# Block means of the values by VectorE sums over features-first values and one transpose, in an attention kernel with two feed-forward stages

## What is computed

```python
k_sum = k.reshape(B, H, nb, 32, D).max(axis=3)       # nb = 24 blocks of 32 tokens
v_sum = v.reshape(B, H, nb, 32, D).mean(axis=3)
scores_l = scale * q @ k^T, kept where |i - j| < 16
scores_s = scale * q @ k_sum^T + log(32)
a = softmax(concat(scores_l, scores_s))
out = a @ concat(v, v_sum)
```

## Time and profile before

| | |
|---|---|
| median of 3 runs | 642.89 us (641.2 to 645.67) |
| span of the profiled execution | 640.1 us |
| TensorE busy (matmul) | 621.3 us, 97% |
| VectorE busy | 446.0 us, 70% |
| ScalarE busy | 262.2 us, 41% |
| GpSimd busy | 145.3 us, 23% |

### The profile page before, as it was taken

One profiled execution on the slowest core, in us unless ns is written; L12 is line 12 of the kernel. 1 busy time (PEld: TensorE's weight loads), 2 busy tenths in 40 slices (PEclk: granted clock), 3 DMA queues, 4 the chain that ended last, 5 costly groups with the idle time before them and its releaser, 6 DMA issues.

```text
span 640.1 us, 9485 instructions
## 1 busy us (share of the span) xinstructions
PE 621.3 (97%) x3072; PEld 519.2 (81%) x3072; DVE 446.0 (70%) x864; ACT 262.2 (41%) x553; POOL 145.3 (23%) x146
## 2 busy tenths in 40 slices
PE   5999998999999999999999989999999999999996
PEld 5999996888888888888888867778888888888885
DVE  4555557966534333345666589999999999999996
ACT  2556553111013111131111374556676666766663
POOL 5344424000003000030000084642222222222220
PEclk9999999999999999999999989999999999999998
DMA  9786744500000000002323310000010000100001
GB/s 215 182 213 179 187 121 175 209 1 0 1 0 0 0 0 0 0 1 98 99 98 100 99 33 0 1 1 0 2 66 0 0 0 0 66 1 0 1 0 66
DMA packets 27096, 35.46 MB, mean 55 GB/s; under 512 B 1984, under 2 KB 19392, under 8 KB 27072
## 3 DMA queue, kind: packets, MB, share of 16 engines
q1 hardware_dynamic: 24672, 33.96, 17.9%
q10 hardware_dynamic: 2400, 1.18, 0.8%
HBM read 30.80 MB, written 3.15 MB: 53 GB/s over the span
## 4 chain that ended last, share of the span: by engine, by line
PE 57%; DVE 34%; issue 6%; ACT 1%; DVEq 1%; DMA 1%; SPq 0%
PE bank L488 21%; PE bank L546 20%; DVE ratio L953 9%; PE bank L443 8%; DVE numer L935 5%; DVE ratio L947 5%; DVE numer L933 5%; DVE ratio L942 5%; DVE hhi L960 4%; PE bank L474 2%; PE bank L461 2%; PE bank L453 2%; PE bank L561 1%; DMA qblk<-qT 1%; DVE hlo L964 0%
## 5 line engine op out<-in xcount | busy, mean ns | idle before, releaser
L488 PE MATMUL bank<-xhi,whi 128*128 (+1 forms) x384 | 150.1, 391 | 1.2 <-DVE wlo L841 1.2
L488 PE MATMUL bank<-xlo,whi 128*128 (+1 forms) x384 | 149.9, 390 | 0.0
L488 PE MATMUL bank<-xhi,wlo 128*128 (+1 forms) x384 | 149.6, 390 | 0.0
L405 POOL TENSOR_TENSOR denom<-denom,habs 128x512 f32<-128x512 f32 (+1 forms) x49 | 62.3, 1271 | 253.0 <-ACT denom L713 253.0
L642 ACT ACTIVATE hsq<-bank 128x512 f32<-128x512 f32 x48 | 28.7, 598 | 218.6 <-PE bank L488 218.6
L488 PEld LDWEIGHTS bank<-xhi,whi 128*128 128x128 f32 x384 | 72.2, 188 | 16.4 <-DVE wlo L841 1.4
L488 PEld LDWEIGHTS bank<-xhi,wlo 128*128 128x128 f32 x384 | 72.3, 188 | 15.1
L488 PEld LDWEIGHTS bank<-xlo,whi 128*128 128x128 f32 x384 | 72.3, 188 | 14.9
L561 PE MATMUL bank<-whi,hhi 128*128 128x512 f32 x192 | 76.8, 400 | 6.5 <-DVE hlo L964 6.5
L561 PE MATMUL bank<-whi,hlo 128*128 128x512 f32 x192 | 76.1, 396 | 0.0
L561 PE MATMUL bank<-wlo,hhi 128*128 128x512 f32 x192 | 75.9, 395 | 0.0
(11 more groups left out here) (69 smaller groups left out, 917.4 us busy)
## 6 DMA issues: line engine op xcount, KB each, us to landing
wraw<-w SPq DMA_DIRECT2D x32, 512.0 KB, 3.8
kraw<-kT SPq DMA_DIRECT2D x8, 384.0 KB, 6.5
qblk<-qT SPq DMA_DIRECT2D x16, 192.0 KB, 3.1
vnat<-v SPq DMA_DIRECT2D x8, 384.0 KB, 5.4
vwin<-v SPq DMA_DIRECT2D x8, 384.0 KB, 4.7
out<-osb SPq DMA_DIRECT2D x12, 256.0 KB, 2.1
vwin<-v SPq DMA_DIRECT2D x16, 88.0 KB, 4.5
vwin<-vsum ACTq DMA_DIRECT2D x8, 144.0 KB
```

What stands on the lines that cost most here:

```text
L405: g.tensor_tensor(denom[:, i, cols], denom[:, i, cols], habs[:, i, cols], ALU.mult).then_inc(q_done, 1)
L488: last = mm(hps[j % 2][:, :], W[a][:, j, kt * P:(kt + 1) * P], X[b][:, kt, bass.ds(CH * c, CH)], start=k == 0, stop=k == 3 * KT - 1)
```

## The change

The means are no longer made by matmuls. The values are loaded a second time features-first, as the keys are (`vT`, 128 features on the partitions, 768 tokens in a row), into `vraw` in place of `vnat`. VectorE sums each 32 tokens with a reduction (`block_sum`) into `vred`, a tile of 128x24. TensorE transposes `vred` once, and ScalarE scales by 1/32 as it copies the result out of PSUM. Both tiles, `vred` and `vsum`, now start at partition 0. The matrix `mean` and what builds it on GpSimd are gone.

`block_sum` stands right behind each `block_max`: whole (24 blocks) for the first two blocks at the start, and in thirds (8 blocks) for block (it+1, s) in the three steps of block (it, s).

```diff
@@ sync
-        def load_vnat(it, s):
-            sp.dma_start(vnat[s][:, :, :], pick(v, it, s).rearrange("(n p) c -> p n c", p=P)).then_inc(vn_in[s], 16)
+        def load_vraw(it, s):
+            sp.dma_start(vraw[s][:, :], pick(vT, it, s)).then_inc(vr_in[s], 16)
...
                 load_q(it + 1, s)
                 load_vwin(*((it, 1) if s == 0 else (it + 1, 0)))
-                sp.wait_ge(vsum_done, n + 1)
-                load_vnat(it + 1, s)
+                sp.wait_ge(vred_done, GPB * (n + 1))
+                load_vraw(it + 1, s)
@@ gpsimd: memset and two affine_select of mean removed
@@ tensor, summary(it, s)
-            pe.wait_ge(vn_in[s], 16 * (it + 1))
+            pe.wait_ge(vred_done, GPB * (n + 1))
             pe.wait_ge(vsum_copied, n)
-            for i in range(S // P):
-                last = mm(vps[KW:COLS, 0:P], mean[:, i, :], vnat[s][:, i, :], start=i == 0, stop=i == S // P - 1)
-            last.then_inc(vsum_done, 1)
+            nc.tensor.transpose(vps[0:NBLK, 0:P], vred[s][:, :], ident[:, :]).then_inc(vsum_done, 1)
@@ scalar, copy_summary
-            a.copy(vsum[s][KW:COLS, :], vps[KW:COLS, 0:P]).then_inc(vsum_copied, 1)
+            a.activation(vsum[s][:, :], vps[0:NBLK, 0:P], ACT.Copy, scale=1.0 / BLOCK).then_inc(vsum_copied, 1)
@@ vector
+        def block_sum(it, s, part, parts, first=False):
+
+            n = B * it + s
+            if part == 0:
+                dve.wait_ge(vr_in[s], 16 * (it + 1))
+                if not first:
+                    dve.wait_ge(vsum_done, n - 1)
+            blocks = NBLK // GPB
+            lo, hi = blocks * part, blocks * (part + parts)
+            d.tensor_reduce(vred[s][:, lo:hi],
+                            vraw[s][:, BLOCK * lo:BLOCK * hi].rearrange("p (n t) -> p n t", t=BLOCK),
+                            AX.X, ALU.add).then_inc(vred_done, parts)
...
                     block_max(it + 1, g // GPB, g % GPB, 1)
+                    block_sum(it + 1, g // GPB, g % GPB, 1)
...
         block_max(0, 0, 0, GPB, first=True)
+        block_sum(0, 0, 0, GPB, first=True)
         make_mask()
...
         block_max(0, 1, 0, GPB, first=True)
+        block_sum(0, 1, 0, GPB, first=True)
         masked(2, 2)
```

More of the change, by code:

```diff
@@ L67, in done, with build @@
     return credits + i + 1
-def build(nc, qT, kT, v, w1, w2, coef_a, coef_b, out):
+def build(nc, qT, kT, vT, v, w1, w2, coef_a, coef_b, out):
     base = 16512
@@ L112, in build @@
     half = FT // 2 * SLOT * 4
-    qblk, kraw, kwin, vwin, vnat = [], [], [], [], []
+    qblk, kraw, kwin, vwin, vraw = [], [], [], [], []
     for s in range(B):
@@ L119, in build @@
         vwin.append(area(f"vwin{s}", [COLS, NW, P]))
-        vnat.append(area(f"vnat{s}", [P, S // P, P]))
+        vraw.append(area(f"vraw{s}", [P, S]))
         assert area.offset <= (W_HI, W_LO)[s] + 2 * half
@@ L126, in build @@
     ident = area("ident", [P, P])
-    mean = area("mean", [P, S // P, NBLK])
-    vsum = [area(f"vsum{s}", [P, P]) for s in range(B)]
+    vred = [area(f"vred{s}", [P, NBLK]) for s in range(B)]
+    vsum = [area(f"vsum{s}", [NBLK, P]) for s in range(B)]
     ksum = [area(f"ksum{s}", [P, NBLK]) for s in range(B)]
@@ L156, in build @@
     k_in = [sem(f"k_in{s}") for s in range(B)]
-    vn_in = [sem(f"vn_in{s}") for s in range(B)]
+    vr_in = [sem(f"vr_in{s}") for s in range(B)]
     vw_in = [sem(f"vw_in{s}") for s in range(B)]
@@ L174, in build @@
     dve_turn = sem("dve_turn")
+    vred_done = sem("vred_done")
     vsum_done = sem("vsum_done")
@@ L256, in _ @@
         load_q(0, 0)
-        load_vnat(0, 0)
+        load_vraw(0, 0)
         sp.wait_ge(cleared, 3)
@@ L261, in _ @@
         load_q(0, 1)
-        load_vnat(0, 1)
+        load_vraw(0, 1)
         sp.dma_start(ca[:, :], coef_a.partition_broadcast(P)).then_inc(coef_in, 16)
@@ L302, in _ @@
         g.memset(ident[:, :], 0.0).then_inc(pool_step, 1)
-        g.memset(mean[:, :, :], 1.0 / BLOCK).then_inc(pool_step, 1)
         for i in range(2):
             g.memset(band[i][:, :], 0.0).then_inc(pool_step, 1)
-        pool.wait_ge(pool_step, 4)
+        pool.wait_ge(pool_step, 3)
         g.affine_select(out=ident[:, :], in_=ident[:, :], compare_op=ALU.not_equal, fill=1.0, base=0,
                         pattern=[[-1, P]], channel_multiplier=1).then_inc(consts, 1)
-        g.affine_select(out=mean[:, :, :], in_=mean[:, :, :], compare_op=ALU.is_ge, fill=0.0, base=0,
-                        pattern=[[P, S // P], [-BLOCK, NBLK]], channel_multiplier=1).then_inc(pool_step, 1)
         for i in range(2):
@@ L316, in _ @@
         pool.wait_ge(consts, 1)
-        pool.wait_ge(pool_step, 7)
-        g.affine_select(out=mean[:, :, :], in_=mean[:, :, :], compare_op=ALU.is_ge, fill=0.0, base=BLOCK - 1,
-                        pattern=[[-P, S // P], [BLOCK, NBLK]], channel_multiplier=-1).then_inc(consts, 1)
+        pool.wait_ge(pool_step, 5)
         for i in range(2):
@@ L526, in attention @@
                     output(it, s, gi, G, g % 2)
-        pe.wait_ge(consts, 4)
+        pe.wait_ge(consts, 1)
         pe.wait_ge(cleared, 3)
@@ L636, in spread_summary @@
             act.dma_start(vwin[s][KW:COLS, :, :],
-                          vsum[s][KW:COLS, :].unsqueeze(1).to_broadcast([NBLK, NW, P])).then_inc(vsum_in[s], 16)
+                          vsum[s][:, :].unsqueeze(1).to_broadcast([NBLK, NW, P])).then_inc(vsum_in[s], 16)
         def relu(n, i):
@@ L776, in make_mask @@
         def make_mask():
-            dve.wait_ge(consts, 4)
+            dve.wait_ge(consts, 3)
             for h in range(2):
@@ L1008, in by_query @@
         return np.ascontiguousarray(features_first(t).reshape(PAIRS, B, P, NW, QW).swapaxes(3, 4))
-    arrays = {"qT": by_query(q), "kT": features_first(k), "v": tokens_first(v),
+    arrays = {"qT": by_query(q), "kT": features_first(k), "vT": features_first(v), "v": tokens_first(v),
               "w1": slots(moe_w_in, moe_w_out), "w2": slots(moe2_w_in, moe2_w_out),
```

## The result

The changed kernel takes 659.75 us (median of 4 runs, 659.52 to 660.97), the kernel before 642.05 us in the same comparison. The ratio is 1.0266, with a 95% interval of 1.0232 to 1.0301: slower by 17.7 us by the medians. The profiled execution took 659.79 us, with a span of 658.0, so 1.8 us lie around the span.

A forecast was written before the change was run, and what follows sets the result against it. TensorE was taken to bound attention; the values' late load would stall blocks: 2.7 + 5 x 3.02 - 1.27 = +16.5 us, plus 1.2 for the clock, together given as +17.6. 642.9 + 17.6 = 660.5 us, range 653 to 667.

The forecast's parts named there:

- T: End of the scores of a block's third group, awaited by SyncE before reloading queries; spacing forecast 14.44 us, before 11.42.
- T to issue: In SyncE's queue, from T to the issue of the values' load, behind query and window loads: 3.33 to 3.36 us.
- The landing, x: Time from issue to landing of the new values' load: 5.0 us, ends 4.3 and 5.7; 6.2 for the first.
- Landing to the next T: Steps from the values' landing through reduction, masked scores, inverse, normalise, transposes and scores to the next T: 6.11 us.
- the clock term: TensorE's standstills in six attention blocks lower its clock: 0.2 us a block, 1.2 in all; at most 0.35 a block.
- The start: First blocks of attention: first T at 13.7, 1.7 us earlier than before; second at 29.0, 2.7 us later.
- The sum: Attention's total shift before the clock: 2.7 + 5 x 3.02 - 1.27 = +16.5 us; with the clock, +17.6.
- a fixed sequence that shifts as a whole: Everything behind attention, from the hidden layer on, moves with the last scores and keeps its length.
- The plain gain: Rival: TensorE stays the bound in attention and keeps 8 x 1.27 = 10.2 us, time 632.7; chance 0.03.
- The light stall (b): Rival: the values' load in attention lands far sooner than its predecessor; 646.8 us at 3.1, 654 at 4.3; chance 0.12.
- 6x - 14.7: Total change in us if all six waited-for loads in attention take x from issue to landing; zero at 2.45.

The follow-up runs named there:

- e9: Changed kernel with 18 filler transposes ahead of the output of each block's second group and 6 more ahead of the third's transposes: 656.94 us, ratio 1.0212.
- e1: Changed kernel with the load of vraw and its wait issued right behind the key load, ahead of SyncE's wait for the scores: 633.41 us, ratio 0.9864.
- e3: Changed kernel with its load unmoved, but VectorE sums all 24 blocks in one reduction in the third step of a block: 632.14 us, ratio 0.9870.
- e2: Changed kernel with the load of vraw issued between the query loads and the window loads: 640.51 us, ratio 0.9988.
- e10: e1 with each reduction of vraw made six times, five of them into unused tiles: 649.55 us in one run.
- e4: Changed kernel with 14 filler transposes into an unused PSUM bank ahead of the output of each block's second group: 658.83 us, ratio 1.0270.

## Why the prediction was right

Direction, place and size came out, but the agreement of 660.5 with 659.75 is closer than the steps deserve: several of them were off and made up for each other. The forecast's own sum has a slip, too: 16.5 + 1.2 is 17.7 and not 17.6. And it put 2.8 us around the span, where the changed kernel has 1.8; most of the rest was the spread of the kernel before, whose median is 642.05 in this comparison and not 642.89.

**T to issue.** 3.33 to 3.36 us forecast; 44.39 to 47.82 is 3.43, and 3.35 in the block before.

**The landing, x.** 5.0 for five blocks and 6.2 for the first. Measured 5.6 for the first, then 5.1, 4.8, 4.9, 5.0 and 5.4. The column of all eight, which answers to the earlier trace rows:

```profile
DMA to landing us min/median/max: 4.8/5.3/7.7
```

Sound. The rows of the keys had left room for something much shorter, and that did not come: median 5.3 for 3,072-byte rows against 5.4 for 512-byte pieces. That agrees with the rule cited from the Trainium skill (DMA: Bandwidth & Descriptors, Specifications), that 512 bytes are enough for line rate, as far as loads that stand behind three others can show it.

**Landing to the next T.** 6.11 us forecast at the high clock and 6.31 with the clock term. Measured 6.40 in the block shown (52.62 to 59.02), and 5.98 in e9 at a clock of 1.00. So the steps were 0.13 too long (the reduction costs 0.33 to the next start and not 0.39, and it starts 0.03 behind the landing and not 0.09), which hid over half of what the clock term lacked. The chain of steps was right, and so was the guess of who waits at the output and at the transposes.

**The clock.** This was the term that was mis-sized. I took 0.2 us a block of at most 0.35, and e9 against the changed kernel shows 0.42. The split was wrong as well. I had let the scores grow by 0.18, from 2.13 to the 2.31 of the very start. But 2.13 is the distance to the next matmul and 2.31 the length of the record, and by records the scores take 2.29 to 2.31 in the steady stretch of the kernel before too. At the low clock they took 2.21 to 2.30: nothing. The four transposes are the price on the path: from their start to that of the scores it is 0.49 us at the high clock (49.13 to 49.62) and 0.90 at the low one (55.81 to 56.71). The rule of the Trainium skill (TensorE: Matmul & The Clock Gate, What's actually happening) pointed to the upper end; the trace and e9 agree with it, and the measured 0.42 lies above that end. The standstills were also shorter than the 3.3 and 0.9 us that I had worked out: 2.42 and 0.34 in the block shown.

**The start.** First T at 13.7 forecast, 14.23 measured, because vraw landed at 8.26 and not at 7.93 and the third scores took 2.49. Second T 29.0 forecast, 29.53 measured, in spite of the shorter x: the load went out 3.65 us behind the first T and not 3.33, and its landing was 6.1 us ahead of the second and not 5.77.

**The sum.** At the first matmul of the hidden layer the changed kernel is 118.99 - 99.69 = 19.3 us behind, where I had 17.7. The second T is 3.2 behind (2.7 forecast). The next five blocks add 17.1 (14.83 us each; 15.1 forecast, and 1.0 for the clock). The last iteration gives back 1.0 of 1.27, as its first matmuls still ran at the low clock. The end of the span is only 17.9 behind: 1.4 us were regained after attention. The trace of the kernel before shows where. Its clock fell behind 380 us, to 0.50 from 381 to 384 us, and that of the changed kernel did not. The same matmul of the second layer is still 19.3 us apart just ahead of it (379.27 and 398.56), and 18.2 just behind it (386.48 and 404.66). So this one fall is 1.1 of the 1.4. A second one in the kernel before (0.50 from 630 to 633 us) left the difference as it was, for in the changed kernel TensorE then stood still for 1.27 us (ahead of the matmul at 651.64), and in the kernel before it did not. Where the clock falls in the layers is an accident, which I had not forecast ("a fixed sequence that shifts as a whole"). It is luck that it made up for the clock term.

**The rivals.** The plain gain was real and sat ready: e1 and e3 have it, once the transfer is in time. The light stall (b) did not come, but its line held: e2 follows it. The six first reductions of e2 start 6.2, 5.1, 5.4, 5.1, 4.9 and 5.0 us behind their T, so by 6x - 14.7 e2 should be about 3 us faster than the kernel before. In its trace the hidden layer starts 3.7 us earlier (at 96.01), and the span is 3.5 shorter. The median is only 0.5 lower, since the profiled execution was the fastest of ten; why the others took longer no trace shows. VectorE's reduction was free, as the earlier trace rows had said, and e10 shows its limit.

## What to carry to other kernels

When a consumer moves to another engine, ask at which step of the loop it now reads, and not only how long it takes; a load that landed six microseconds ahead of its use (57.8 and 63.83 us in the kernel before) comes too late when its use moves three steps ahead, and its issue is held by whatever its queue waits for before it. Follow the new wait through the queue of the engine that waits: the cost here was not the reduction (0.33 us, covered) but everything behind it. A change that loses can be one moved line from a gain, so price the placement apart from the work.

## What the chip showed

- With a standstill of TensorE of 2.4 to 3.0 us in each block of 14.8, the granted clock was 0.73 from 29.5 to 103.3 us, although TensorE was busy for about 80% of it. With the standstills mostly filled by useless transposes (e9, up to 1.6 us left) it was 1.00, and the kernel was faster for the added work.
- At the lower level the four transposes went from 0.65 to 1.11 us and the sixteen output matmuls from 0.69 to 1.12, but the scores stayed at 2.2 to 2.3. Their weight loads take 0.37 us each at either level, which may be what sets their pace; that was not tried.
- A filler of 1.69 us in standstills of 2.3 to 3.4 was not enough (e4): the clock came back from 0.77 to 0.87 only.
- The length of a standstill alone does not say whether the clock falls. The second layer has the same standstill in both kernels: 2.10 us ahead of the matmul at 379.27 before, 2.12 ahead of the one at 398.56 now. Before, the clock was 0.50 from 381 to 384 us; now it was 1.00 from 399 to 404.
